# GpSimd's copies for a pair of heads ahead of its sums and splits, and the transfers in another order, in a fused attention and two-layer kernel

## Chip, core and metric

One core of a Trainium2 chip runs the whole kernel. The metric is the device time of one execution in microseconds.

## What is computed

The reference, cut to what matters (B, H, S, D = 2, 8, 768, 64; blocks of 32 keys, a window of 16):

```python
k_sum = k.reshape(B, H, nb, block, D).max(axis=3)
v_sum = v.reshape(B, H, nb, block, D).mean(axis=3)
scores_l = scale * q @ k^T            # kept where |i - j| < 16
scores_s = scale * q @ k_sum^T + log(32)
a = softmax(concat([scores_l, scores_s]))
x = a @ concat([v, v_sum])            # reshaped to 1536 x 512
h = x @ w_in                          # 512 -> 1024
solu = h * softmax(h); ln = layernorm(solu) * g_ln
x = ln @ w_out                        # 1024 -> 512
h = x @ w2_in                         # 512 -> 2048
out = where(h > 0, h, exp(min(h, 0)) - 1) @ w2_out
```

## The kernel before, in words

The kernel is written engine by engine, with semaphores between them; each engine runs its instructions in the order written, and every load is issued on the DMA queue of SyncE (SP).

**Attention stage.** The 16 heads go by pairs, 8 pairs of 6 units of 128 queries (48 units). For a pair, TensorE turns k (L881, `prep_k`) and q (L894, `prep_q`) with the identity; for a unit it computes scores against the neighbouring 96 keys (L910) and 24 block maxima (L918); VectorE adds the mask and finds the maximum (L694), ScalarE takes the exponential (L510), TensorE turns the probabilities (L927, L928, `turn_probs`), they are copied, and `attend` (L943) multiplies them by `vw`. Attend runs three units behind the scores, turning the probabilities two. After three attended units VectorE normalises them, and TensorE turns the result (L955) for the next stage.

`vw` holds three slots (VS = 3), one for each pair in turn. A slot has for each of 12 sub-blocks of 64 queries: 64 rows of v and 2 x 16 halo rows, and 24 rows of block means. The DMA queue loads the 64 own rows and part of the halo (`load_v`, L294 and L298). GpSimd copies the other halo rows from the neighbouring sub-block (`fill_halo`, L435), and spreads the block means over the 12 sub-blocks of both heads (`spread_means`, L444, two copies). The first attend of a pair waits for both.

The block means come from `vblocks` (two slots, four loads of 256 KB each, `load_vblocks`, L315): GpSimd adds halves until 64 columns are left (`block_means`, L408), and scales (L412); one call serves two pairs (four heads), so there are four calls (MEANS = 4). For the first one VectorE adds the first half (L728).

GpSimd also splits the weights of the first layer into high and low parts: `split_win` (L416, L418), four quarters of 512 KB, loaded by `load_win` (L319); and `split_wout`, four quarters, loaded by `load_wout` (L322). The first layer's products (L866 to L868) need all of win split, its second product (L1023 to L1025) all of wout.

k and q have four slots each (RAWS = 4; L277 and L284, two transfers of 192 KB per pair, one for each head, 64 numbers or 256 B a row; v is 384 KB and 8 KB). A load waits for its slot: v of pair n for attend group 6(n - 2) (that is, pair n - 3 attended), k and q for the turning of pair n - 4, vblocks c for the means of c - 2. A wait on SP holds all that is written behind it.

**Later stages.** x @ w_in row tile by row tile with softmax and layer norm (L748 to L808), then ln @ w_out; w2_in is loaded once the last scores are done, and w2_out after the first layer's products. The two products of the second layer (L866 to L868 and L1067 to L1069) fill the rest of the time from about 270 us on.

Of the kernel before, what the change touches and what calls it, by code (L numbers as in the profile page):

```python
# [25 lines left out]
P = 128  # L26


def fused_layers_kernel(nc, q, k, v, w_in, g_ln, w_out, w2_in, w2_out, out):
# [8 lines left out]
    PAIRS = B * H // 2  # L38
# [18 lines left out]
    KD = DM // P  # L57
# [11 lines left out]
    with ExitStack() as ctx:  # L69
# [57 lines left out]
        RING, VS = 4, 3  # L127

        HPM = P // BLOCK
        MEANS = B * H // HPM  # L130
# [32 lines left out]
        def sem(name):  # L163
            return ctx.enter_context(nc.semaphore(name))
# [11 lines left out]
        gcol_loaded = sem("gcol_loaded")  # L176
# [9 lines left out]
        win_hi_done, win_split, wout_hi_done, wout_split = (  # L186
            sem("win_hi_done"), sem("win_split"), sem("wout_hi_done"), sem("wout_split"))
# [19 lines left out]
        for g in range(GROUPS):  # L207
# [7 lines left out]
            else:  # L215
                ROWS_AND_TURNS[-1][1].extend(range(c, c + KF))
        assert [m for m, _ in ROWS_AND_TURNS] == list(range(TILES))
        assert [c for _, cs in ROWS_AND_TURNS for c in cs] == list(range(KF * GROUPS))
        TURNS = KF * GROUPS
        OUT_LAG = 2  # L220
# [34 lines left out]
        def v_landed(n):  # L255

            return 16 * (2 * (n // VS + 1) + (2 if n == PAIRS - 1 else 0))
# [11 lines left out]
        def _(sp):  # L269
            def pair_of_heads(x, n):  # L270
                return x[2 * n:2 * n + 2].rearrange("h (t p) d -> p t h d", p=P)

            def load_k(n):
                if n >= RAWS:
                    sp.wait_ge(kv_in_psum, n - RAWS + 1)
                for h in range(2):
                    sp.dma_start(kraw[:, n % RAWS, :, h * D:(h + 1) * D],  # L277
                                 pair_of_heads(kf, n)[:, :, h, :]).then_inc(k_loaded[n % RAWS], 16)

            def load_q(n):  # L280
                if n >= RAWS:
                    sp.wait_ge(q_in_psum, n - RAWS + 1)
                for h in range(2):
                    sp.dma_start(qraw[:, n % RAWS, :, h * D:(h + 1) * D],  # L284
                                 pair_of_heads(qf, n)[:, :, h, :]).then_inc(q_loaded[n % RAWS], 16)

            def load_v(n):

                s = n % VS
                if n < VS:  # L290
                    sp.wait_ge(zeros_ready, 1)
                else:
                    sp.wait_ge(attn_done, T * (n - VS + 1))
                sp.dma_start(vw[HALO:2 * HALO, s, :, 0, 0:D],  # L294
                             vf[2 * n:2 * n + 2, 0:HALO, :].rearrange("h i d -> i h d")).then_inc(v_loaded[s], 16)
                if n < PAIRS - 1:
                    rows = v_rows[2 * n * S + HALO:2 * (n + 1) * S + HALO, :].rearrange("(j i) d -> i j d", i=SUB)
                    sp.dma_start(vw[2 * HALO:LOCAL, s, :, :, 0:D].rearrange("i h j d -> i (h j) d"), rows).then_inc(v_loaded[s], 16)  # L298
                else:
                    rest = S - HALO - (SUBS - 1) * SUB  # L300
                    rows = v_rows[2 * n * S + HALO:(2 * n + 1) * S + HALO, :].rearrange("(j i) d -> i j d", i=SUB)
                    sp.dma_start(vw[2 * HALO:LOCAL, s, 0, :, 0:D], rows).then_inc(v_loaded[s], 16)
                    rows = vf[2 * n + 1, HALO:S - rest, :].rearrange("(j i) d -> i j d", i=SUB)
                    sp.dma_start(vw[2 * HALO:LOCAL, s, 1, 0:SUBS - 1, 0:D], rows).then_inc(v_loaded[s], 16)
                    sp.dma_start(vw[2 * HALO:2 * HALO + rest, s, 1, SUBS - 1, 0:D], vf[2 * n + 1, S - rest:S, :]
                                 ).then_inc(v_loaded[s], 16)

            def load_vblocks(c):

                if c >= 2:  # L310
                    sp.wait_ge(vmean_ready, c - 1)
                for i in range(HPM):
                    b0 = (HPM * c + i) * NB
                    b1 = min(b0 + QUAD, B * H * NB)
                    sp.dma_start(vblocks[i * QUAD:i * QUAD + b1 - b0, c % 2, :], v_blocks[b0:b1, :]  # L315
                                 ).then_inc(vblocks_loaded[c % 2], 16)

            def load_win(i):
                sp.dma_start(win_raw[:, i, :], w_in[i * P:(i + 1) * P, :]).then_inc(win_loaded[i], 16)  # L319

            def load_wout(i):
                sp.dma_start(wout_raw[:, 2 * i:2 * i + 2, :],  # L322
                             w_out[2 * i * P:(2 * i + 2) * P, :].rearrange("(k p) n -> p k n", p=P)
                             ).then_inc(wout_loaded[i], 16)
# [4 lines left out]
            load_k(1)  # L329
            load_v(0)  # L330
            load_q(1)
            load_v(1)
            load_vblocks(1)
            load_k(2)
            load_q(2)
            for n in range(PAIRS):
                if n + 2 < PAIRS:
                    load_v(n + 2)
                if n + 3 < PAIRS:
                    load_k(n + 3)  # L340
                    load_q(n + 3)
                if n < KD:
                    load_win(n)
                if 1 <= n and n + 1 < MEANS:
                    load_vblocks(n + 1)
                if n >= KD:
                    load_wout(n - KD)
                if n == KD:
                    sp.dma_start(gcol[:, :], g_ln.rearrange("(f p) -> p f", p=P),
                                 allow_slow_non_contiguous=True).then_inc(gcol_loaded, 16)  # L350

            sp.wait_ge(scores_in_psum, UNITS)
            sp.wait_ge(q_in_psum, PAIRS)
# [18 lines left out]
        def _(pool):  # L372
# [27 lines left out]
            def block_means(c):  # L400

                x, width = vblocks[:, c % 2, :], BLOCK * D // 2
                pool.wait_ge(vblocks_loaded[c % 2], 16 * HPM * (c // 2 + 1))
                if c == 0:
                    pool.wait_ge(first_half_summed, 1)
                    width //= 2
                while width >= D:
                    pool.tensor_tensor(x[:, 0:width], x[:, 0:width], x[:, width:2 * width], ALU.add).then_inc(vsum_step, 1)  # L408
                    vsteps[0] += 1
                    pool.wait_ge(vsum_step, vsteps[0])  # L410
                    width //= 2
                pool.tensor_scalar(vmean[:, c, :], x[:, 0:D], 1.0 / BLOCK, None, ALU.mult).then_inc(vmean_ready, 1)  # L412
                pool.wait_ge(vmean_ready, c + 1)

            def split(raw, hi, lo, hi_done, done, n):
                pool.tensor_copy(hi, raw).then_inc(hi_done, 1)  # L416
                pool.wait_ge(hi_done, n + 1)
                pool.tensor_tensor(lo, raw, hi.bitcast(F32), ALU.subtract).then_inc(done, 1)  # L418

            def split_win(i):  # L420
                pool.wait_ge(win_loaded[i], 16)
                split(win_raw[:, i, :], win_hi[:, i, :], win_lo[:, i, :], win_hi_done, win_split, i)
# [6 lines left out]
            def fill_halo(n):  # L429

                s = n % VS
                pool.wait_ge(v_loaded[s], v_landed(n))
                if n == 0:
                    pool.wait_ge(zeros_ready, 2)
                pool.tensor_copy(vw[0:2 * HALO, s, :, 1:SUBS, :],  # L435
                                 vw[SUB:LOCAL, s, :, 0:SUBS - 1, :]).then_inc(halo_filled, 1)
                pool.wait_ge(halo_filled, n + 1)

            def spread_means(n):

                s, c = n % VS, n // (HPM // 2)
                for h in range(2):
                    i = (2 * n + h) % HPM
                    pool.tensor_copy(vw[LOCAL:KEYS, s, h, :, 0:D],  # L444
                                     vmean[i * QUAD:i * QUAD + NB, c, None, :].broadcast_to([NB, SUBS, D])
                                     ).then_inc(means_spread, 1)
                    pool.wait_ge(means_spread, 2 * n + h + 1)

            block_means(0)
            fill_halo(0)  # L450
            spread_means(0)
            block_means(1)
            for n in range(PAIRS):
                if n < KD:
                    split_win(n)
                    pool.wait_ge(win_split, n + 1)
                if n + 1 < PAIRS:
                    fill_halo(n + 1)
                    spread_means(n + 1)
                if 1 <= n and n + 1 < MEANS:  # L460
                    block_means(n + 1)
            for i in range(KF // 2):
                split_wout(i)

            for g in range(GROUPS):
                pool.wait_ge(factors_ready, g + 1)
                for t in range(TG - pool_rows(g), TG):
                    i = (TG * g + t) % LNS
# [641 lines left out]
```

## Time and profile before

| | |
|---|---|
| median of 3 runs | 542.33 us (538.64 to 547.3) |
| profiled execution | 542.89 us, its span 541.1 us |
| mean granted TensorE clock | 0.972 of full speed |
| TensorE busy (matmuls) | 497.5 us, 92% of the span |
| VectorE, ScalarE, GpSimd busy | 232.1, 212.6, 127.5 us |
| moved by the DMA engines | 29.83 MB |

The span runs from the first to the last instruction of the profiled execution. Times in a timeline are microseconds from the span's start. A busy TensorE isn't TensorE at its peak, since its matmuls overlap and their ends are modelled.

### The profile page before, as it was taken

What the parts mean: (1) busy time and instruction counts of PE and PEld (TensorE: products, weight loads), DVE (VectorE), ACT (ScalarE), POOL (GpSimd) and SP (SyncE); (2) the same over time, 40 slices, a digit from 0 to 9 for tenths busy, and PEclk for the clock granted to TensorE, in tenths of its full rate; (3) what the DMA queues carried; (4) which work ended last, traced back from release to release, by engine and by line L of the source; (5) the groups of instructions that cost most, each with busy time, mean ns of one, the idle gap of its engine ahead of it and who ended that gap; (6) DMA issues with size and microseconds to landing.
All of it is one profiled execution on the core that took longest, in us unless ns stands there. A gap on an engine that the chain in (4) does not pass through costs nothing.

```text
span 541.1 us, 8560 instructions
## 1 busy us (share of the span) xinstructions
PE 497.5 (92%) x3312; PEld 417.2 (77%) x3312; DVE 232.1 (43%) x623; ACT 212.6 (39%) x433; POOL 127.5 (24%) x121
## 2 busy tenths in 40 slices
PE   3848669889699999999999999999999999999997
PEld 2636557667588989889988888888888888888886
DVE  2334525661686255355346555433333332323231
ACT  2434626671566254435464343323222223222222
POOL 2658396560012001102335545200000000000000
PEclk9987958999899999999999999999999999999999
DMA  9993936507000000008000000002000001000002
GB/s 187 216 233 89 232 97 129 149 13 302 0 0 2 0 1 1 1 1 310 2 0 1 0 1 1 1 0 79 0 1 0 1 0 68 10 0 0 0 0 78
DMA packets 45766, 29.83 MB, mean 55 GB/s; under 512 B 39596, under 2 KB 39596, under 8 KB 44716
## 3 DMA queue, kind: packets, MB, share of 16 engines
q1 hardware_dynamic: 45732, 29.37, 21.1%
q8 instruction: 23, 0.38, 0.3%
q14 instruction: 11, 0.09, 0.1%
HBM read 26.21 MB, written 3.15 MB: 54 GB/s over the span
## 4 chain that ended last, share of the span: by engine, by line
PE 81%; SPq 6%; POOL 3%; DVE 3%; DMA 3%; ACT 2%; issue 2%; POOLq 0%; DVEq 0%
PE bank L866 12%; PE bank L868 12%; PE bank L867 11%; PE bank L1069 8%; PE bank L1067 8%; PE bank L1068 8%; PE bank L1023 4%; PE bank L1025 4%; PE bank L1024 3%; PE bank L943 3%; SPq L284 3%; DMA win_raw<-in_w_in 3%; PE bank L910 2%; PE bank L1009 2%; SPq L277 1%
## 5 line engine op out<-in xcount | busy, mean ns | idle before, releaser
L627 ACT ACTIVATE ex<-bank 128x512 f32<-128x512 f32 x48 | 28.7, 598 | 127.9 <-PE bank L868 127.9
L868 PE MATMUL bank<-yt_lo,w2in_hi 128*128 (+1 forms) x192 | 74.7, 389 | 0.0
L867 PE MATMUL bank<-yt_hi,w2in_lo 128*128 (+1 forms) x192 | 74.7, 389 | 0.0
L1067 PE MATMUL bank<-w2out_hi,g_hi 128*128 128x512 f32 x192 | 74.7, 389 | 0.0
L1068 PE MATMUL bank<-w2out_lo,g_hi 128*128 128x512 f32 x192 | 74.7, 389 | 0.0
L866 PE MATMUL bank<-yt_hi,w2in_hi 128*128 (+1 forms) x192 | 74.7, 389 | 0.0
L1069 PE MATMUL bank<-w2out_hi,g_lo 128*128 128x512 f32 x192 | 74.7, 389 | 0.0
L844 DVE TENSOR_SCALAR ex<-ex 128x512 f32<-128x512 f32 x48 | 21.6, 450 | 116.4 <-ACT ex L627 116.4
L849 DVE TENSOR_TENSOR g_lo<-gf,g_hi 128x512 fp32r<-128x512 f32 x48 | 46.5, 969 | 35.9 <-ACT g_hi L635 35.9
L510 ACT ACTIVATE se<-se,nm 128x120 f32<-128x120 f32 x96 | 32.6, 387 | 49.7 <-DVE nm L694 49.7
L635 ACT ACTIVATE g_hi<-gf 128x512 fp32r<-128x512 f32 x48 | 30.3, 632 | 49.0 <-DVE gf L846 49.0
L1023 PE MATMUL bank<-lnt_hi,wout_hi 128*128 128x384 f32 x128 | 45.6, 356 | 1.2 <-DVE lnt_lo L803 1.2
L694 DVE CUSTOM_DVE_ANT_0 se<-bank,mask 128x120 f32<-128x120 f32 x96 | 23.1, 279 | 54.7 <-PE bank L918 54.7
L943 PE MATMUL bank<-vw,pt 120*64 120x65 f32 x384 | 24.8, 256 | 20.5 <-POOL vw L444 19.8
L866 PE MATMUL bank<-win_hi,xt_hi 128*128 128x512 f32 x96 | 38.9, 405 | 4.7 <-DVE su L764 4.7
L1025 PE MATMUL bank<-lnt_lo,wout_hi 128*128 128x384 f32 x128 | 43.1, 337 | 0.0
L1024 PE MATMUL bank<-lnt_hi,wout_lo 128*128 128x384 f32 x128 | 42.9, 335 | 0.0
L469 POOL TENSOR_SCALAR ln<-ln,st 128x1024 f32<-128x1024 f32 x10 | 12.5, 1260 | 125.1 <-DVE st L790 125.1
L1068 PEld LDWEIGHTS bank<-w2out_lo,g_hi 128*128 128x128 f32 x192 | 36.0, 188 | 7.6
L868 PEld LDWEIGHTS bank<-yt_lo,w2in_hi 128*128 128x128 f32 x192 | 36.0, 188 | 7.6
L1069 PEld LDWEIGHTS bank<-w2out_hi,g_lo 128*128 128x128 f32 x192 | 36.0, 188 | 7.5
L867 PEld LDWEIGHTS bank<-yt_hi,w2in_lo 128*128 128x128 f32 x192 | 36.0, 188 | 7.5
(102 smaller groups left out, 883.6 us busy)
## 6 DMA issues: line engine op xcount, KB each, us to landing
w2in_raw<-in_w_in SPq DMA_DIRECT2D x1, 4096.0 KB, 12.4
w2out_raw<-in_w_out SPq DMA_DIRECT2D x4, 1024.0 KB, 9.5
vblocks<-in_v SPq DMA_DIRECT2D x15, 256.0 KB, 6.1
kraw<-in_k SPq DMA_DIRECT2D x16, 192.0 KB, 4.8
qraw<-in_q SPq DMA_DIRECT2D x16, 192.0 KB, 4.4
out<-osb SPq DMA_DIRECT2D x12, 256.0 KB, 2.1
vw<-in_v SPq DMA_DIRECT2D x7, 384.0 KB, 5.0
win_raw<-in_w_in SPq DMA_DIRECT2D x4, 512.0 KB, 5.7
```

Of the source, the lines that this page charges most:

```text
L510: last = act.activation(se[:, s, h, :], se[:, s, h, :], ACT.Exp, scale=-1.0, bias=nm[:, s, h:h + 1])
L849: dve.tensor_tensor(g_lo[:, j % GS, :], gf[:, :], g_hi[:, j % GS, :].bitcast(F32), ALU.subtract).then_inc(glo_ready, 1)
L866: pe.matmul(acc, ah, bh, start=(i == 0), stop=False)
L867: pe.matmul(acc, al, bh, start=False, stop=False)
L868: last = pe.matmul(acc, ah, bl, start=False, stop=(i == n - 1))
L943: last = pe.matmul(psO[i * SUB:(i + 1) * SUB, c0:c0 + D1], pt[0:KEYS, u % 2, q0:q0 + SUB], vw[0:KEYS, v, h, 2 * t + i, :], start=True, sto ...
L1023: pe.matmul(dst, wout_hi[:, f, cols], lnt_hi[:, f, :], start=(f == 0), stop=False)
L1024: pe.matmul(dst, wout_lo[:, f, cols], lnt_hi[:, f, :], start=False, stop=False)
L1025: last = pe.matmul(dst, wout_hi[:, f, cols], lnt_lo[:, f, :], start=False, stop=(f == KF - 1))
L1067: pe.matmul(dst, g_hi[:, j % GS, cols], w2out_hi[:, j, :], start=(j == 0), stop=False)
L1068: pe.matmul(dst, g_hi[:, j % GS, cols], w2out_lo[:, j, :], start=False, stop=False)
L1069: last = pe.matmul(dst, g_lo[:, j % GS, cols], w2out_hi[:, j, :], start=False, stop=(j == KJ - 1))
```

## The change

GpSimd's program and the order of SP's loads are written out anew; no instruction of any other engine changes, and neither does the number or shape of any instruction or transfer.

```diff
             load_q(1)
+            load_k(2)
             load_v(1)
+            load_q(2)
             load_vblocks(1)
-            load_k(2)
-            load_q(2)
-            for n in range(PAIRS):
-                if n + 2 < PAIRS:
-                    load_v(n + 2)
-                if n + 3 < PAIRS:
-                    load_k(n + 3)
-                    load_q(n + 3)
-                if n < KD:
-                    load_win(n)
-                if 1 <= n and n + 1 < MEANS:
-                    load_vblocks(n + 1)
-                if n >= KD:
-                    load_wout(n - KD)
-                if n == KD:
-                    sp.dma_start(gcol[:, :], ...)
+            load_v(2)
+            load_k(3)
+            load_q(3)
+            load_win(0)
+            for n in range(VS, PAIRS):
+                load_v(n)
+                if n - 2 < KD:
+                    load_win(n - 2)
+                if n + 1 < PAIRS:
+                    load_k(n + 1)
+                    load_q(n + 1)
+                if n % 2 == 1 and n // 2 + 1 < MEANS:
+                    load_vblocks(n // 2 + 1)
+                if n >= 6:
+                    load_wout(n - 6)
+            sp.dma_start(gcol[:, :], ...)
+            load_wout(2)
+            load_wout(3)
...
+            def finish_v(n):
+                fill_halo(n)
+                spread_means(n)
+
+            def finish_win(i):
+                split_win(i)
+                pool.wait_ge(win_split, i + 1)
+
             block_means(0)
-            fill_halo(0)
-            spread_means(0)
+            finish_v(0)
+            finish_v(1)
             block_means(1)
-            for n in range(PAIRS):
-                if n < KD:
-                    split_win(n)
-                    pool.wait_ge(win_split, n + 1)
-                if n + 1 < PAIRS:
-                    fill_halo(n + 1)
-                    spread_means(n + 1)
-                if 1 <= n and n + 1 < MEANS:
-                    block_means(n + 1)
+            finish_v(2)
+            finish_win(0)
+            finish_win(1)
+            finish_v(3)
+            block_means(2)
+            finish_v(4)
+            finish_win(2)
+            finish_v(5)
+            block_means(3)
+            finish_v(6)
+            finish_win(3)
+            finish_v(7)
             for i in range(KF // 2):
                 split_wout(i)
```

## Rows read from the trace of the kernel before

**Rows 1.** The page: busy tenths and granted clock by slices; the chain by line.

```profile
PE   3848669889699999999999999999999999999997
...
PEclk9987958999899999999999999999999999999999
...
PE bank L866 12%; PE bank L868 12%; PE bank L867 11%; PE bank L1069 8%; PE bank L1067 8%; PE bank L1068 8%; PE bank L1023 4%; PE bank L1025 4%; PE bank L1024 3%; PE bank L943 3%; SPq L284 3%; DMA win_raw<-in_w_in 3%; PE bank L910 2%; PE bank L1009 2%; SPq L277 1%
```

**Rows 2.** Waits of TensorE, 0 to 130 us: total, times, longest.

```profile
PE bank L943 <- POOL vw L444: 19.8, 3, 9.3
PE bank L881 <- DMA kraw<-in_k: 7.3, 2, 4.8
```

**Rows 3.** Timeline of TensorE: start, duration, instructions, in brackets the idle time before.

```profile
20.16 0.70 PE L943 MATMUL bank<-vw,pt 120*64 120x65 f32 x8 [2.57 <-POOL vw L444]
...
32.84 0.27 PE L928 MATMUL bank<-ident,se 128*120 128x128 f32 x1
42.43 0.70 PE L943 MATMUL bank<-vw,pt 120*64 120x65 f32 x8 [9.32 <-POOL vw L444]
...
53.45 0.27 PE L928 MATMUL bank<-ident,se 128*120 128x128 f32 x1
53.66 0.45 PE L943 MATMUL bank<-vw,pt 120*64 120x65 f32 x8
...
71.76 0.70 PE L943 MATMUL bank<-vw,pt 120*64 120x65 f32 x8 [7.90 <-POOL vw L444]
...
86.37 0.45 PE L943 MATMUL bank<-vw,pt 120*64 120x65 f32 x8
...
96.50 0.45 PE L943 MATMUL bank<-vw,pt 120*64 120x65 f32 x8
...
104.92 0.39 PE L943 MATMUL bank<-vw,pt 120*64 120x65 f32 x5 [0.75 <-issue]
...
107.65 0.45 PE L943 MATMUL bank<-vw,pt 120*64 120x65 f32 x8
...
131.26 0.45 PE L943 MATMUL bank<-vw,pt 120*64 120x65 f32 x8
```

**Rows 4.** Timeline of GpSimd (POOL).

```profile
24.17 5.43 POOL L408 TENSOR_TENSOR vblocks<-vblocks 128x1024 f32<-128x1024 f32 x5 [4.16 <-DMA vblocks<-in_v]
...
35.52 1.04 POOL L416 CAST win_hi<-win_raw 128x1024 fp32r<-128x1024 f32 x1 [5.46 <-DMA win_raw<-in_w_in]
...
39.04 1.36 POOL L435 COPY vw<-vw 32x1430 f32<-32x1430 f32 x1
40.47 1.71 POOL L444 COPY vw<-vmean 24x768 f32<-24x768 f32 x2
43.09 1.04 POOL L416 CAST win_hi<-win_raw 128x1024 fp32r<-128x1024 f32 x1 [0.91 <-DMA win_raw<-in_w_in]
...
64.85 1.04 POOL L416 CAST win_hi<-win_raw 128x1024 fp32r<-128x1024 f32 x1 [9.10 <-DMA win_raw<-in_w_in]
...
157.61 1.74 POOL L469 TENSOR_SCALAR ln<-ln,st 128x1024 f32<-128x1024 f32 x1 [40.27 <-DVE st L790]
```

**Rows 5.** Stretches: busy time by engine, then granted clock, DMA share, GB/s.

```profile
0.00:24.17 24.17, 12.46 (x130) 9.81 (x134) 6.24 (x28) 7.98 (x17) 9.32 (x25) 1.00 1.07 200
24.17:35.52 11.35, 8.94 (x131) 6.89 (x130) 6.14 (x30) 5.88 (x16) 5.48 (x7) 1.00 1.03 229
35.52:43.09 7.57, 0.66 (x12) 0.57 (x12) 0.00 (x0) 0.00 (x0) 6.38 (x6) 0.59 1.06 236
...
52.50:70.30 17.80, 10.52 (x195) 8.01 (x195) 9.48 (x45) 9.48 (x26) 8.16 (x9) 0.92 1.02 203
```

**Rows 6.** Timeline of the DMA queue (SPq): v of pairs 3 and 4, win 2.

```profile
31.90 0.34 SPq L294 DMA_DIRECT2D vw<-in_v  x1
...
52.52 0.32 SPq L294 DMA_DIRECT2D vw<-in_v  x1
...
56.76 0.84 SPq L319 DMA_DIRECT2D win_raw<-in_w_in  x1
```

More of the change, by code:

```diff
@@ L331, in _ @@
             load_q(1)
+            load_k(2)
             load_v(1)
+            load_q(2)
             load_vblocks(1)
-            load_k(2)
-            load_q(2)
-            for n in range(PAIRS):
-                if n + 2 < PAIRS:
-                    load_v(n + 2)
-                if n + 3 < PAIRS:
-                    load_k(n + 3)
-                    load_q(n + 3)
-                if n < KD:
-                    load_win(n)
-                if 1 <= n and n + 1 < MEANS:
-                    load_vblocks(n + 1)
-                if n >= KD:
-                    load_wout(n - KD)
-                if n == KD:
-                    sp.dma_start(gcol[:, :], g_ln.rearrange("(f p) -> p f", p=P),
-                                 allow_slow_non_contiguous=True).then_inc(gcol_loaded, 16)
+            load_v(2)
[13 more added lines that the diff above has]
+                    load_wout(n - 6)
+            sp.dma_start(gcol[:, :], g_ln.rearrange("(f p) -> p f", p=P),
+                         allow_slow_non_contiguous=True).then_inc(gcol_loaded, 16)
+            load_wout(2)
+            load_wout(3)
             sp.wait_ge(scores_in_psum, UNITS)
```

## Prediction

> **What bounds the kernel now.** I read the page's slices first, then who waits for whom on TensorE, then the timelines of TensorE, GpSimd and the DMA queue side by side over the attention stage. In the slices TensorE is at 9 tenths nearly everywhere after the tenth slice (13.5 us each), and its holes lie in the third, fifth and sixth; the granted clock is low there or in the slice behind them, and in the chain by line the weight transfer win_raw has 3% of the span beside TensorE's own lines [rows 1]. So what can be won without touching the products lies in the first 130 us.
>
> There TensorE waits 19.8 us in three pieces for L444, the spread of block means, and 7.3 us in two for the first transfers of k [rows 2]. I number TensorE's attend groups (L943, eight matmuls) A0 to A47, six to a pair; A6, A12, A18 are the first of pairs 1, 2, 3. A0 starts at 20.16 after 2.57 us of waiting. A6 starts at 42.43 after 9.32 us; the probabilities for it were turned from 32.84. A18 starts at 71.76 after 7.90 us [rows 3]. GpSimd tells why. After the sums of vblocks 1 it waited 5.46 us for win_raw 0, split it, and only then copied halo and means of pair 1 (39.04 to 42.18), which had long been loadable. The same happened before A18: 9.10 us of waiting for win_raw 2, at 64.85 [rows 4]. The wait that ends last is thus a transfer of weights that the attention doesn't need, standing ahead of a 3.1 us copy in GpSimd's program. Its root is the DMA queue: its v transfer waits for attend groups, and one held it until 52.52, with win 2 issued behind it at 56.76 [rows 6].
>
> **The clock.** A matmul group of A takes 0.70 us just after each hole and 0.45 us later [rows 3]: the granted clock is at its 1.2 GHz level after a hole and comes back to 2.4. Six attend slots at full clock take 96.50 - 86.37 = 10.13 us (A24 to A30) [rows 3]. I take this as the price of a pair when nothing is late.
>
> **The change part by part.**
>
> GpSimd's program. The work is the same: no instruction is added or removed, only their order. So the first question is whether each copy of halo and means is ready before its pair. One pair of them costs 1.36 + 1.71 and some 0.1 of waits, 3.15 us; a sum of blocks 5.43 for the halvings, 6.0 us with the scaling and the waits (the first call is shorter, and the same in both); a split of win 3.5 us (35.52 to 39.04) [rows 4].
>
> The queue's program. The transfers are the same too, q and k still in two parts of 256 B rows each. Ahead of vblocks 1 now stand k 2 and q 2; from n = 3 on, win stands before k and q instead of behind them; vblocks 2 and 3 are issued at n = 3 and 5, the latter one v wait later. v of pair n still waits for the same attend group as before, as do k and q behind it. Nothing that waits for TensorE has moved ahead of something needed sooner.
>
> When things land. A pair of k or of q is 0.39 MB, of v 0.40, vblocks 1.05, a quarter of win 0.52. By 24.17 the DMA engines had moved 24.17 x 0.200 = 4.83 MB, when vblocks 1 landed with 4.47 MB ordered up to its end; at 35.52 and 43.09 win 0 and win 1 landed with 7.43 and 9.22 moved against 6.97 and 8.68 ordered [rows 4, 5]. So a transfer lands when about 0.45 MB more than its place in the order have moved. In the new order, at the same rates: v 1 (place 3.82) at 21.4, vblocks 1 (5.26) at 28.0, v 2 (5.66) at 29.8, win 0 at 35.4; v 3 is issued at 31.90 as before, being bound to A5 [rows 6], and lands at 37.2, win 1 at 39.4, vblocks 2 about 46.
>
> GpSimd against TensorE, then. Pair 1's copies start when v 1 is in, end at 24.6, and are needed at 33.05 (32.84 plus the 0.21 that lie between the rows at 53.45 and 53.66) [rows 3]. Sums of vblocks 1: 28.0 to 34.0. Pair 2's copies end 37.2, needed at A12. If nothing waits, A12 = 33.05 + 10.13 = 43.2, A18 = 53.3, A24 = 63.4, A30 = 73.6, A36 = 83.7. Win 0 and 1: to 44.2; pair 3: 47.4 against 53.3; sums 2: 53.3; pair 4: 56.5 against 63.4 (v 4, freed by A11 at 42, lands at about 50). Each has 6 us or more to spare.
>
> For the later transfers I take the 0.203 MB/us of the stretch 52.5 to 70.3 [rows 5], from 45.5 on when the queue would be empty. From v 4 to the end of vblocks 3 are 4.47 MB, plus 0.45: landed at 45.5 + 24.2 = 69.7. Sums 3 end 75.7 and pair 6 at 78.9, against 83.7: 4.8 us to spare, the tightest place. k 7 lands about 74 and is wanted about 80. win 3 and pair 7 follow, to 85.5 against 93.9, and the four splits of wout by about 100. These are moved behind nothing critical: in the trace of before GpSimd is done with wout so early that it then waits 40.27 us until 157.61 [rows 4], so 100 is early enough even for a stage that starts 23 us sooner.
>
> The sum. Hole before A6: 42.43 - 33.05 = 9.38. Half clock behind it: A6 to A12 took 53.66 - 42.43 = 11.23, less 10.13 = 1.10. A12 to A18: 71.76 - 53.66 = 18.10, less 10.13 = 7.97. A18 to A24: 86.37 - 71.76 = 14.61, less 10.13 = 4.48 [rows 3]. Together 22.9 us, of which 5.6 are clock. A0's wait and the two for k at the start stay: nothing ahead of them changes. What follows A30 is the same work, so it moves as a block. The profiled execution took 542.89 with a span of 541.1; 542.9 - 22.9 = **520.0**. The median of the runs is 542.33, 0.6 lower, within their spread of 538.64 to 547.3; I keep 520.
>
> Bounds of what the trace doesn't show. (a) Four pairs in a row without a hole: A30 to A36 took 107.65 - 96.50 = 11.15 us because of one gap of 0.75 that has no releaser but TensorE's own queue [rows 3]; with such a gap in each of four pairs the gain is 4 us smaller, 524. (b) After attention the slices show one more low slice of clock, a dip from 1.0 to about 0.87 over a slice of 13.5 us; were it spared, some 2 us more would be gained, and another 2 if the clock rose sooner after A0, 516. The nearest row for (a) is the neighbour of the one I use; I take none, since the other pairs at full clock ran without it.
>
> **The rivals.**
>
> *The transfers become the bound (R1).* Without holes TensorE uses a pair every 10.13 us, and a middle pair now orders 1.19 MB of k, q and v, 0.52 of weights and half of 1.05: 2.2 MB, at 0.203 some 11 us. The queue's lead therefore shrinks by 1 us a pair. Pair 6 is late if the rate falls under 4.92 / (83.7 - 9.2 - 45.5) = 0.170 MB/us. Against it: no stretch of rows 5 is below 0.200. At 0.150 the sums would start at 78.3, TensorE would wait 3.8 us, and the clock would drop once more, at the 4.5 us that it cost after A18: 528.
>
> *One copy is still late (R2).* If a transfer of win takes the 8.0 us from issue that win 2 took before (56.76 to some 64.8 [rows 4, 6]), win 1 lands at 41 rather than 39.4, and pair 3 still has 4 us. Only two such delays in the same stretch open a hole of a few us with its clock: 526. For it: sums of blocks still stand between the copies. Together with R1 I give these 523 to 532.
>
> *The clock stays low (R3), the slower side.* One mechanism: TensorE in this stage is a chain of short groups with gaps between them, and if the granted clock does not stay up without the old stops, every pair costs at least the 14.61 us of A18 to A24. A36 would come at 33.05 + 5 x 14.61 = 106.1, 1.5 before the old one; the stretch from there to the last attend group (131.26 - 107.65 = 23.6 us [rows 3]) would take 1.44 times as long, 10.4 more: about 552. It decides once more than half of the stage runs at 1.2 GHz. Against it: in the eighth to tenth slices the clock is at 9 while the same groups run without a hole [rows 1]. The Trainium skill, "TensorE: Matmul & The Clock Gate", section "A second HAM failure mode: psum-queue depth-cycling", describes just this: small idle times between matmul groups, often enough, make the clock swing between its two levels. By that rule 552 would be the time, by the rows 520; the rows from A24 to A36 speak against the rule here.
>
> *The order changes nothing (R4).* Halo and means could be late for v itself instead of for win. v 1 would have to land after 33; it was landed before the sums of vblocks 1 started at 24.17, so this needs 9 us of delay. Time 540.
>
> **How the numbers follow.** Forecast (with its bounds 516 to 524) 0.72; R1 and R2 together 0.18, at 523 to 532; R3 0.04; R4 0.03; the rest, 0.03, a gain larger than the bounds. The range 515 to 530 leaves out R3, R4 and the end of R1 and R2. Two per cent is about what a measurement of this kernel can tell from no change: 531.5. Below it lie the forecast, the larger gain and most of R1 and R2: 0.90; within 2%: 0.06; slower by more: 0.04, nearly all R3.
>
> **What the changed profile should show.** No wait of TensorE for L444 but the first, 2.6 us; A6 about 33, A12 43, A18 53, A30 74, and the last attend group about 108; the clock's slices at 9 from the third to the tenth; GpSimd waiting for vblocks 1 about 4 us after pair 1's copies, and no more than 1 or 2 us for win; the queue moving over 0.2 MB/us nearly without a break until 75. What would make me wrong: a wait of GpSimd for vblocks 3 that reaches A36, a wait for k in the later pairs, or groups of A at 0.70 us where there is no hole.

## The result, and the profile after

The changed kernel takes 517.29 us (median of 4, 516.36 to 517.76) against 544.51 of the kernel before (538.64 to 547.3): a ratio of 0.9532, interval 0.9443 to 0.9622. (The ratios, here and below, leave out executions more than 1.5% above the fastest of their kernel, like the one at 547.3; the medians don't.) Measured beside the experiments below, the kernel before had medians of 541.4 to 542.0. The changed kernel's profiled execution took 517.02 with a span of 515.2, against 542.89 and 541.1: 25.9 us less in the span.

The page's slices (each 12.9 us now), to be held against [rows 1]: the low slices of the attention stage are gone. The ninth, with 6 tenths, lies behind that stage and has its like in the kernel before (the eleventh). No digit of the granted clock is under 9.

```profile
PE   3798998969999999999999999999999999999997
...
PEclk9999999999999999999999999999999999999999
```

A 9 can hide a low clock, in two ways. At the start the row has 9 while groups of A still take 0.70 us (below): up to the clock's first rise the row reads as full, so there I go by the lengths of the groups. And behind the attention stage the dip that showed as an 8 in the kernel before is still there. TensorE waits 4.16 us in both, until 139.46 before and 113.63 now, and the clock is at 0.50 in the microseconds behind it; the slices only fall otherwise. These are stretches (columns as in [rows 5]), of the kernel before and of the changed one:

```profile
140.00:141.00 1.00, 1.00 (x4) 0.76 (x3) 0.96 (x5) 0.65 (x1) 0.00 (x0) 0.50 0.00 0
...
114.00:115.00 1.00, 1.00 (x3) 0.79 (x3) 0.96 (x4) 0.47 (x1) 0.00 (x0) 0.50 0.00 0
```

Waits of TensorE in its first 110 us, against [rows 2]: of the three waits for the spread of the means (L448 now) one is left, and the two for k at the start stand as they did.

```profile
PE bank L896 <- DMA kraw<-in_k: 7.3, 2, 4.6
...
PE bank L958 <- POOL vw L448: 2.4, 1, 2.4
```

Timeline of TensorE, attend groups (L958 now), against [rows 3]: A0, A2, A6, A12, A18, A24, A30, A36, A42 and A47.

```profile
19.83 0.70 PE L958 MATMUL bank<-vw,pt 120*64 120x65 f32 x8 [2.40 <-POOL vw L448]
...
24.83 0.46 PE L958 MATMUL bank<-vw,pt 120*64 120x65 f32 x8
...
31.06 0.45 PE L958 MATMUL bank<-vw,pt 120*64 120x65 f32 x8
...
41.23 0.45 PE L958 MATMUL bank<-vw,pt 120*64 120x65 f32 x8
...
51.98 0.45 PE L958 MATMUL bank<-vw,pt 120*64 120x65 f32 x8
...
61.60 0.45 PE L958 MATMUL bank<-vw,pt 120*64 120x65 f32 x8
...
71.73 0.45 PE L958 MATMUL bank<-vw,pt 120*64 120x65 f32 x8
...
81.86 0.45 PE L958 MATMUL bank<-vw,pt 120*64 120x65 f32 x8
...
91.85 0.45 PE L958 MATMUL bank<-vw,pt 120*64 120x65 f32 x8
...
105.44 0.45 PE L958 MATMUL bank<-vw,pt 120*64 120x65 f32 x8
```

A47 came at 105.44 instead of 131.26: 25.8 us sooner, and from there to the end 409.8 us pass in both kernels. The whole gain lies in the attention stage. By stretches between these rows (before, after):

| stretch | before | after | gain |
|---|---|---|---|
| start to A0 | 20.16 | 19.83 | 0.3 |
| A0 to A6 | 22.27 | 11.23 | 11.0 |
| A6 to A12 | 11.23 | 10.17 | 1.1 |
| A12 to A18 | 18.10 | 10.75 | 7.4 |
| A18 to A24 | 14.61 | 9.62 | 5.0 |
| A24 to A30 | 10.13 | 10.13 | 0.0 |
| A30 to A36 | 11.15 | 10.13 | 1.0 |
| A36 to A47 | 23.61 | 23.58 | 0.0 |

GpSimd's timeline, against [rows 4]. It shows the new order, the copies of pairs 1 to 4 before they are wanted, and the two long waits behind the first spread: 4.46 us for vblocks 1, and 6.32 us for vblocks 3, behind which pair 6's copies end at 79.00. No wait for win is left.

```profile
20.64 1.37 POOL L439 COPY vw<-vw 32x1430 f32<-32x1430 f32 x1 [0.95 <-DMA vw<-in_v]
22.07 1.71 POOL L448 COPY vw<-vmean 24x768 f32<-24x768 f32 x2
28.23 5.45 POOL L412 TENSOR_TENSOR vblocks<-vblocks 128x1024 f32<-128x1024 f32 x5 [4.46 <-DMA vblocks<-in_v]
...
35.63 1.71 POOL L448 COPY vw<-vmean 24x768 f32<-24x768 f32 x2
...
45.94 1.71 POOL L448 COPY vw<-vmean 24x768 f32<-24x768 f32 x2
...
55.12 1.71 POOL L448 COPY vw<-vmean 24x768 f32<-24x768 f32 x2
...
69.90 5.45 POOL L412 TENSOR_TENSOR vblocks<-vblocks 128x1024 f32<-128x1024 f32 x5 [6.32 <-DMA vblocks<-in_v]
...
77.29 1.71 POOL L448 COPY vw<-vmean 24x768 f32<-24x768 f32 x2
```

The stretch from 45.5 us, where the prediction began its reckoning, to the landing of vblocks 3, against the last row of [rows 5]: the DMA engines are busy throughout (share 1.02) at 208 GB/s.

```profile
45.50:69.80 24.30, 22.61 (x432) 17.71 (x427) 16.06 (x83) 18.46 (x50) 16.95 (x17) 1.00 1.02 208
```

The queue's v transfers of pairs 3 and 4, against [rows 6], are issued 1.3 and 10.4 us sooner, since the attend groups that free them come sooner.

```profile
30.60 0.43 SPq L294 DMA_DIRECT2D vw<-in_v  x1
...
42.10 0.43 SPq L294 DMA_DIRECT2D vw<-in_v  x1
```

### The profile page after: what moved, and what is told of

The parts are those of the page before. It is cut to its first block, busy times and chain, and to the rows that moved or that the text cites. A ratio compares the mean times of both kernels' runs of the same rounds, so it can differ in the third digit from the quotient of the medians.

```text
span 515.2 us, 8560 instructions
## 1 busy us (share of the span) xinstructions
PE 487.8 (95%) x3312; PEld 409.9 (80%) x3312; DVE 231.2 (45%) x623; ACT 212.2 (41%) x433; POOL 127.7 (25%) x121
## 4 chain that ended last, share of the span: by engine, by line
PE 88%; DVE 3%; issue 2%; ACT 2%; POOL 2%; DMA 1%; SPq 1%; DVEq 0%; POOLq 0%
PE bank L881 12%; PE bank L882 12%; PE bank L883 12%; PE bank L1082 8%; PE bank L1083 8%; PE bank L1084 8%; PE bank L1038 4%; PE bank L1040 4%; PE bank L1039 4%; PE bank L958 3%; PE bank L925 3%; PE bank L942 2%; PE bank L1024 2%; PE bank L970 1%; DMA vblocks<-in_v 1%
## 5 line engine op out<-in xcount | busy, mean ns | idle before, releaser
L1082 PEld LDWEIGHTS bank<-w2out_hi,g_hi 128*128 128x128 f32 x192 | 36.1, 188 | 7.5
L881 PEld LDWEIGHTS bank<-yt_hi,w2in_hi 128*128 128x128 f32 x192 | 36.0, 188 | 7.5
```

What stands on the lines that cost most here:

```text
L881: pe.matmul(acc, ah, bh, start=(i == 0), stop=False)
L1082: pe.matmul(dst, g_hi[:, j % GS, cols], w2out_hi[:, j, :], start=(j == 0), stop=False)
```

## The experiments

### Which of the two orders did it

Two kernels take one half of the change each. In the first, the block of loads is that of before; in the second, GpSimd's is.

```diff
 e1_gpsimd_only: the changed kernel
-            load_k(2)   ... the new order of loads
+            load_v(1)   ... the loads as before the change
 e2_queue_only: the kernel before
-            load_v(1)   ... its order of loads
+            load_k(2)   ... the changed one
```

Expected of the first:

> Only GpSimd's new order, with the transfers in the order of before. My theory (GpSimd's order was the cause; the transfers' order is worth little): every copy is still ready in time. Copies of pair 1 end near 23, sums 1 near 30, pair 2 near 33, win 0 and 1 near 46.5, pair 3 near 49.6 against A18 at 52, pair 4 near 58.7 against 61.6, the later ones earlier still. A47 at 105 to 106, the time within 1 us of the changed kernel: 516 to 519. Rival (both parts are needed): k, q or win come late in the old order, TensorE waits at pair 4 or 5 with its clock falling behind, 521 to 530.

It took 519.39 us against 541.98 of the kernel before, measured beside it: ratio 0.9589 (0.9519 to 0.9659). A47 came at 107.64. So GpSimd's order alone gives 22.6 us. The time is 0.4 over my theory's bound and A47 1.6 us later than it had; A0 came at 21.16, 1.3 us later than in the changed kernel. The rows of its GpSimd timeline run about 1 us behind the expected ones: pair 3's copies end at 50.6, a wait of 4.21 for win 1 stands before them, and TensorE doesn't wait for them.

```profile
43.92 1.04 POOL L416 CAST win_hi<-win_raw 128x1024 fp32r<-128x1024 f32 x1 [4.21 <-DMA win_raw<-in_w_in]
...
48.90 1.71 POOL L444 COPY vw<-vmean 24x768 f32<-24x768 f32 x2
```

Expected of the second:

> Only the new order of the transfers, with GpSimd's program of before. My theory: it makes things worse. Win 0 at 35.4 still stands ahead of pair 1's copies, so A6 stays near 42; and the sums of vblocks 3, loaded later now, stand ahead of win 3 and pair 4's copies: vblocks 3 lands near 77, sums to 83, win 3 to 86.5, pair 4's copies near 89.6, A24 near 90 after a hole of some 17 us, against 86.37 before. The hole before A18 shrinks to 0 to 3 us. Time 543 to 553. Rival (the transfers' order is what gave the gain, since weights come earlier): 525 to 535.

It took 547.59 us: ratio 1.0103 (1.0067 to 1.0139): about 1% slower than before, and clear of 1. TensorE's timeline has the three holes where they were expected: A6 as late as before, A18 with a small one, A24 with the long one (13.51 us where I had said some 17), as GpSimd waited 11.69 us for vblocks 3 and then split win 3 ahead of pair 4's copies.

```profile
41.91 0.70 PE L947 MATMUL bank<-vw,pt 120*64 120x65 f32 x8 [10.59 <-POOL vw L448]
...
65.45 0.45 PE L947 MATMUL bank<-vw,pt 120*64 120x65 f32 x8 [1.61 <-POOL vw L448]
...
89.73 0.70 PE L947 MATMUL bank<-vw,pt 120*64 120x65 f32 x8 [13.51 <-POOL vw L448]
```

GpSimd's timeline of the same kernel has the wait that leads to the last of them:

```profile
76.89 5.41 POOL L412 TENSOR_TENSOR vblocks<-vblocks 128x1024 f32<-128x1024 f32 x5 [11.69 <-DMA vblocks<-in_v]
```

The same order of transfers thus costs 5.6 us with one program on GpSimd and gains a little with the other: its cost is not its own, but that of what waits behind it.

### Is it the weights alone that stood in the way

```diff
 in GpSimd's loop of the kernel before
-                if n < KD:
-                    split_win(n)
-                    pool.wait_ge(win_split, n + 1)
                 if n + 1 < PAIRS:
                     fill_halo(n + 1)
                     spread_means(n + 1)
+                if n < KD:
+                    split_win(n)
+                    pool.wait_ge(win_split, n + 1)
```

> The kernel before, with one swap in GpSimd's loop: the copies of pair n + 1 stand ahead of the split of win n; sums of blocks and transfers as before. My theory: both holes shrink, but the sums, still ahead of the copies, leave small ones. Pair 1's copies end near 33.2 against A6 at 31 to 33 (hole up to 2 us), pair 3's near 55.6 against 53.3 (hole 2), pair 4's near 68 against 66 (hole 2), later ones in time. Time 523 to 530. Rival (the wait for win was all of it): within 1 us of the changed kernel, 516 to 519.

527.32 us, ratio 0.9702 (0.9639 to 0.9766): 14.7 us gained by one swap. The kernel with all of GpSimd's new order and the same transfers took 519.39, so the rest of that order, which takes the sums from in front of the copies too, is worth 7.9 us more. In TensorE's timeline the hole before A6 is 0.47 us, that before A18 4.62 (2 expected), and behind it the groups are at 0.70 us:

```profile
33.45 0.45 PE L943 MATMUL bank<-vw,pt 120*64 120x65 f32 x8 [0.47 <-POOL vw L444]
...
58.03 0.70 PE L943 MATMUL bank<-vw,pt 120*64 120x65 f32 x8 [4.62 <-POOL vw L444]
...
72.54 0.45 PE L943 MATMUL bank<-vw,pt 120*64 120x65 f32 x8
```

A18 to A24 takes 14.51 us. The hole that I had expected before A24 was not there: TensorE had been slow for so long that pair 4's copies, done at 70.5, caught up. So the losses of two pairs can't simply be added.

### The share of the clock

```diff
 the kernel before, attend, first group of pairs 1 and 3
+                    if n in (1, 3):
+                        pe.wait_ge(xn_ready, w)
+                    for _ in range({1: WARM1, 3: WARM3}.get(n, 0)):
+                        pe.matmul(psO[:, 2 * TG * D1:2 * TG * D1 + 96], ident[:, :], ident[:, 0:96], start=True, stop=True)
                     pe.wait_ge(halo_filled, n + 1)
```

> The kernel before, with 105 and 90 matmuls of 128 by 96 that nobody reads ahead of TensorE's two long waits for the copies of pairs 1 and 3 (and the wait for the normalised heads moved ahead of them). It tells the clock's share of the gain from the holes' own. My theory (5.6 us of the gain are half clock behind the holes): the holes stay in place, A6 near 42.4, but groups of A stay at 0.45 us; A6 to A12 and A18 to A24 take 10.1 instead of 11.2 and 14.6; time 5 to 6 us under before, 536 to 539. Rival (the slow groups behind a hole are caught up later because something else bounds them, or the clock falls nonetheless): within 2 us of before.

A miss of mine: 560.07 us, ratio 1.0321 (1.0258 to 1.0384). The fillers took 22.72 us where the hole was to be 9.3. I had taken 0.083 us for one from the pace of the transposes; it is 22.72 / 105 = 0.216. The trace says why. Each such product of 4-byte numbers stands in it as two matmuls (the 105 and 90 of the program add 390 to TensorE's 3312), while a transpose of the same numbers stands as one. The other half of the theory shows even here: behind the fillers A6 to A12 and A18 to A24 take 9.27 us each, at 0.45 us a group.

```profile
31.81 22.72 PE L939 MATMUL bank<-ident 128*128 128x96 f32 x202
```

With 40 and 33 of them:

> The keep-clock kernel again: the fillers took 0.216 us each, not the 0.083 I had reckoned with, so 105 and 90 of them were 22.7 and 20.3 us long and made the holes longer. Now 40 and 33, some 8.6 and 7.1 us. Theory (half clock behind the holes is 5 to 6 us of the gain): A6 near 42.4, A6 to A12 and A18 to A24 about 9.3 to 10.1, time 535 to 538. Rival (the clock's share is caught up): within 2 us of before.

Median 538.11 us against 541.41: ratio 0.9952 (0.9921 to 0.9983), 3.3 us. The profiled execution, at 535.0 the fastest of ten, shows the case in full: the fillers keep TensorE busy for 9.14 us, A6 stays late at 42.70, all groups are at 0.45, and the granted clock is 1.00 until TensorE's wait behind the attention stage.

```profile
33.63 9.14 PE L939 MATMUL bank<-ident 128*128 128x96 f32 x80
42.70 0.45 PE L948 MATMUL bank<-vw,pt 120*64 120x65 f32 x8
...
51.97 0.45 PE L948 MATMUL bank<-vw,pt 120*64 120x65 f32 x8
...
70.31 0.45 PE L948 MATMUL bank<-vw,pt 120*64 120x65 f32 x8
...
80.50 0.45 PE L948 MATMUL bank<-vw,pt 120*64 120x65 f32 x8 [0.86 <-POOL vw L445]
```

A6 to A12 takes 9.27 us there, less than the 10.13 of a steady pair, for which I take it that the other engines caught up in the hole. A18 to A24 takes 10.19, 4.4 less than before. So the clock's share is real: 1.96 + 4.42 = 6.4 us by these two stretches in this execution, the catching up included, and 3.3 in the median. The mean granted clock is 0.997 here and 0.981 to 0.993 in the other nine, so in them it was low for longer, somewhere; they have no trace. The wait itself is most of the loss, as reckoned.

### The price of a hole

Into the changed kernel, between `block_means(2)` and `finish_v(4)`, go 3 or 6 additions that nobody reads:

```diff
+            for _ in range(3):      # 6 in the second
+                pool.tensor_tensor(vblocks[:, 0, 0:1024], vblocks[:, 0, 1024:2048],
+                                   vblocks[:, 0, 1024:2048], ALU.add).then_inc(vsum_step, 1)
+                vsteps[0] += 1
+                pool.wait_ge(vsum_step, vsteps[0])
```

> The changed kernel with three more additions of 128 by 1024 numbers (2.37 us each, into a part of the block buffer that nobody reads any more) on GpSimd between the third sums and pair 4's copies: 7.1 us. It measures the slack there and the price of a short hole. In the changed kernel pair 4's copies ended at 56.8 and A24 came at 61.6, so 4.8 us are free. Theory: a hole of 2.3 to 2.6 us before A24, no fall of the clock behind so short a hole, time 2.5 us over the changed kernel, 519 to 520. Rival (a short hole costs clock too): 522 to 525.

Median 520.06 us, 518.44 to 524.9: the median is as the theory had it, the highest as the rival. The trace is of that highest one. A24 waits 3.37 us, and a granted clock of 0.50 follows:

```profile
64.71 0.70 PE L963 MATMUL bank<-vw,pt 120*64 120x65 f32 x8 [3.37 <-POOL vw L448]
...
79.40 0.45 PE L963 MATMUL bank<-vw,pt 120*64 120x65 f32 x8
```

A24 to A30 takes 14.69 us, 4.6 more than a steady pair: the clock costs more than the hole. The executions of 518.44 and 519.14 us had a mean clock of 0.997, that of the changed kernel's profiled one, so theirs didn't fall at this place. Whether they had the same hole and chance decided, or a shorter one, isn't shown, as they have no trace. (The additions took 1.89 us each, and the sums of vblocks 2 had started 1.7 us later than in the changed kernel. Together they put the end of pair 4's copies from 56.8 to 64.5, 7.6 us, while A24 came 3.1 us later: 4.5 us of it were free, near the 4.8 that I had reckoned with.)

> The same with six additions, 14.3 us: 9.5 us beyond the slack. Theory (a long hole costs itself and half clock behind it, 1 to 5 us as in the kernel before): a hole of 9.5 us before A24, groups of A at 0.70 us behind it, 11 to 15 us over the changed kernel, 528 to 532. Rival (waiting engines catch up behind the hole, as A6 to A12 did in 9.27 us when fillers kept the clock): 526 to 527.

Median 528.48 us, 528.2 to 529.73: 11.4 over the 517.1 of the changed kernel as measured for the next section, within the theory. Pair 4's copies ended at 69.3 and A24 came at 69.58, 8.0 us behind the changed kernel's 61.60, A30 at 84.22 (14.64 later). The wait next to A24 reads only 4.74 us, for behind a gap of 1.33, at 51.46, the clock had already fallen once, and slow groups used up a part of the hole:

```profile
51.46 0.49 PE L975 MATMUL bank<-ident,xn 128*128 128x128 f32 x3 [1.33 <-DVE xn L735]
...
69.58 0.70 PE L963 MATMUL bank<-vw,pt 120*64 120x65 f32 x8 [4.74 <-POOL vw L448]
```

Its stretch behind that gap has a granted clock of 0.58:

```profile
52.00:60.00 8.00, 8.00 (x105) 6.25 (x105) 3.36 (x19) 4.37 (x11) 7.44 (x8) 0.58 0.98 231
```

### What the transfers' order is worth

The changed kernel and the one with the old transfers again, side by side on one chip:

> The changed kernel itself, on the same chip as the next two, so that one can be held against the other. Both theories: 516 to 518, the last attend group about 105.

517.12 us (516.04 to 517.72), ratio 0.9563 (0.9529 to 0.9598).

> GpSimd's new order with the old transfers, beside the changed kernel on the same chip. In the first run it was 2.1 us over the changed kernel's median of another chip job; there 1.7 us of it was a wait of TensorE for q and 1.3 us a later A0, before which nothing differs. Theory A (the transfers' order is worth the wait for q, 1 to 2 us, and A0 was chance): 1 to 2.5 us above the changed kernel here, with the wait for q again. Theory B (worth nothing): within 0.5 us.

Median 521.72 us, ratio 0.9637 (0.9583 to 0.9692): 4.6 above it, or 3.3 without the highest execution, 526.46; more than either theory had. The intervals of the ratios just overlap, but five of the six executions lie above all six of the changed kernel. A part of the theory fell with the traces. The wait of 1.7 us for q, of which it spoke, was that for the first q of all, ahead of A0, where the two orders are still the same; behind A0 neither profiled execution has one. What there is instead are gaps of about 1 us with no releaser:

```profile
50.64 0.49 PE L966 MATMUL bank<-ident,xn 128*128 128x128 f32 x3 [0.81 <-issue]
...
65.86 0.30 PE L929 MATMUL bank<-ks,qt 64*64 64x24 f32 x5 [1.19 <-issue]
```

Of the 1.96 us by which this profiled execution is longer than the changed kernel's beside it, 0.9 come after A47, where the two programs are the same: 410.7 us against 409.8, and over 112 to 120 us, behind TensorE's wait of 4.16, its granted clock is 0.57 on average against 0.79 in the changed kernel's first profile. That dip was longer by chance.

To see which part of the order matters, each half of it was undone in the changed kernel:

```diff
 e11_queue_later_part
-            load_k(2); load_v(1); load_q(2); load_vblocks(1)
+            load_v(1); load_vblocks(1); load_k(2); load_q(2)
 e12_queue_early_part: from v of pair 3 on
-            v n, win n-2, k n+1, q n+1; vblocks 3 with n = 5
+            v n, k n+1, q n+1, win n-2; vblocks 3 with n = 4
```

> The changed kernel, with the early transfers (through v of pair 2) in the old order: v 1, vblocks 1, k 2, q 2. Only the later part of the queue's order is new. In the last call the old order as a whole gave 521.7 with a spread of 517 to 526, the new one 517.1 with 516 to 518. Theory A (it is the later part, win ahead of k and q and vblocks 3 later, that steadies the time): 516 to 518.5 here. Theory B (it is k 2 and q 2 early): 519 to 523.

518.81 us (517.99 to 521.35), ratio 0.9592 (0.9564 to 0.9619): 0.3 over Theory A's bound, and just under Theory B's. In its profiled execution (517.99) A47 came at 104.94, 0.5 sooner than in the changed kernel, so the attention stage lost nothing there; the dip behind A47 was the longer one.

> The other half: k 2 and q 2 early, the later transfers in the old order (k and q ahead of win, vblocks 3 one v wait sooner). Theory A: 519 to 523, as widely spread as with the whole old order. Theory B: 516 to 518.5.

523.89 us, 517.37 to 528.54, ratio 0.9625 (0.9579 to 0.9671). The pair speaks for Theory A, that the later part of the order is what steadies the time, though the intervals of the ratios overlap. The profiled execution (525.11 us) shows how one becomes long. A gap of 2.36 us without a releaser stands in pair 2, and A12 to A18 then takes 16.33 us:

```profile
42.48 0.45 PE L958 MATMUL bank<-vw,pt 120*64 120x65 f32 x8
...
47.37 0.37 PE L942 MATMUL bank<-ident,se 128*120 128x128 f32 x1 [2.36 <-issue]
...
47.89 0.70 PE L958 MATMUL bank<-vw,pt 120*64 120x65 f32 x8
...
58.81 0.45 PE L958 MATMUL bank<-vw,pt 120*64 120x65 f32 x8
```

In the stretches the clock falls within the gap (0.74 as its mean) and is at 0.50 behind it; the groups of A are at 0.70 us up to 55.77, and 55 to 58 has a mean of 0.77. That makes some 10 us at the lower level. The columns are as in [rows 5].

```profile
45.00:47.30 2.30, 0.01 (x1) 0.00 (x0) 0.00 (x0) 0.18 (x1) 2.24 (x2) 0.74 1.27 199
47.30:50.00 2.70, 2.63 (x32) 1.79 (x33) 0.58 (x5) 1.22 (x3) 2.50 (x4) 0.50 0.64 128
50.00:55.00 5.00, 5.00 (x59) 3.99 (x58) 2.71 (x13) 2.45 (x8) 4.60 (x6) 0.50 1.01 234
```

What the gap waits for isn't shown. But the DMA rows hold a trail. The page has two queues that it calls "instruction", q8 and q14; q8 moves 23 packets of 0.02 MB in a whole execution. Some gaps of TensorE in the attention stage stand in some traces and not in the others, and aren't waits for the spread of the means. From A0 to 110 us all traces together have twelve of 0.45 us or more: the 2.36 above and one of 0.46 in the same trace, 0.81 and 1.19 above, 0.51 in the changed kernel, 0.75 in the kernel before, 1.63 and 0.45 in the first half-change, 0.81 in the second, 0.79 in the next experiment, 0.57 in the kernel with 40 and 33 fillers, 1.33 in the one with six additions. All twelve end 2.3 to 3.1 us after a packet of q8 has started, and six of them stand at the same place of the program, the transposes of xn just ahead of A18. For the 0.45, which ended at 59.65, the packet shows in the stretch from 56.8 to 57.0:

```profile
q8 instruction: 1, 0.02, 40.6%
```

Most packets of q8 are followed by no gap. This fits code that arrives late, behind data that fill the DMA engines, but no run here took the data away, so it stays argued. Why the old later order should bring such gaps more often stays open too.

### One step further

What TensorE's first wait ends on is GpSimd's chain of sums, halo and spread. ScalarE is idle for 1.5 us between 15.7 and 17.9 (0.43 and 1.09), and can take the halo copy of pair 0, which GpSimd then leaves out:

```diff
 in ScalarE's loop, behind copy_k(1)
+                if u == 1:
+                    act.wait_ge(v_loaded[0], v_landed(0))
+                    act.wait_ge(zeros_ready, 2)
+                    act.activation(vw[0:2 * HALO, 0, :, 1:SUBS, :], vw[SUB:LOCAL, 0, :, 0:SUBS - 1, :],
+                                   ACT.Copy).then_inc(halo0_filled, 1)
```

> The changed kernel, with the halo copy of pair 0 done by ScalarE behind its first copy of k, so that GpSimd goes from the first means to their spreading. Theory (what TensorE's first wait ends on is GpSimd's chain of sums, halo and spread): A0 about 1.3 us sooner, wait 1.1 instead of 2.4, and all behind it moves along: 1 to 1.4 us under the changed kernel, 515.0 to 516.5. Rival (the clock's rise or the next wait eats it, or ScalarE's exponentials come later): no difference.

517.67 us (515.29 to 522.75) beside 517.12: no difference that counts, and a wider spread. The mechanism is there, A0 comes at 18.50, 1.3 us sooner. But in this execution (519.65 us) the clock was still low when it had risen in the changed kernel: the sixth group still took 0.67 us, and A6 came at 32.52 instead of 31.06.

```profile
18.50 0.70 PE L962 MATMUL bank<-vw,pt 120*64 120x65 f32 x8 [1.08 <-POOL vw L446]
...
30.68 0.67 PE L962 MATMUL bank<-vw,pt 120*64 120x65 f32 x8
32.52 0.45 PE L962 MATMUL bank<-vw,pt 120*64 120x65 f32 x8
```

That need not come of the earlier A0: with the 40 and 33 fillers A0 came at 19.64 and the groups were as slow for as long. Three of the six executions, from 515.29 to 517.00, are as fast as the changed kernel or faster; whether the clock rose early in them isn't shown, as they have no trace. No version of these beats the changed kernel.

## Why the prediction was right

The forecast was 520.0, in the range 515 to 530; the time is 517.3.

*What bounds the kernel.* Right, and tested from both sides: taking the split of win from in front of the copies gives 14.7 us, moving the copies ahead of the later sums as well gives 22.6, both with the old transfers; the new transfers without GpSimd's new order lose 5.6.

*GpSimd against TensorE.* The reckoned times (what TensorE's grid allowed aside) came within 0.9 us everywhere: pair 1's copies ended at 23.8 (24.6 reckoned), sums 1 at 34.2 (34.0), pair 2 at 37.3 (37.2), win 0 and 1 at 44.4 (44.2), pair 3 at 47.7 (47.4), pair 4 at 56.8 (56.5), vblocks 3 landed at 69.9 (69.7), pair 6's copies at 79.0 (78.9), pair 7's at 85.8 (85.5). The rate taken for the later transfers, 0.203 MB/us, is near the 0.208 measured. One landing was off by more: vblocks 2 came at 47.4 rather than about 46, which cost nothing, since GpSimd was ready for it only at 47.7. And "6 us or more to spare" was too much: pairs 2, 3 and 4 had 3.9, 4.3 and 4.8 us, as TensorE's grid ran some 2 us ahead of the reckoned one.

*The sum.* The mechanism held and the terms of the second hole were sized well: 7.97 + 4.48 = 12.45 against 7.35 + 4.99 = 12.34 measured; so was the clock behind the first, 1.10 against 1.1. Too small was the term of the hole before A6: A0 to A6 got shorter by 11.0 us rather than 9.4, because the clock rose at A2 (24.83) and not at A4. That is luck of the two profiled executions and no work of the change: among kernels that are the same up to there, the groups were at 0.70 us up to A1 (the 105 fillers), A3 (before, and the swap) and A5 (the 40 fillers). A0 itself came 0.3 sooner, and the gap of 0.75 us between A30 and A36, which I had left in the block that moves, was gone, 1.0 us. The clock's rise and the gap are in the bounds that I gave, the one in (b), the other the reverse of (a). Together these make up the 2.9 us by which the span shrank more than forecast (25.9 against 22.9); by medians measured side by side the gain is 24.3. The other part of (b) didn't come: the low clock behind the attention stage wasn't spared, though its digit went from 8 to 9, and A47 to the end took 409.8 us in both.

*The rivals.* R1: pair 6 had 81.86 - 79.00 = 2.9 us to spare rather than 4.8, since TensorE came 1.8 us sooner; the transfers are not the bound, but they are near. R2 didn't come true in either profile of the changed kernel. R3: the clock stayed up through the whole stage with gaps of up to 0.9 us in each pair, so the Trainium skill's "TensorE: Matmul & The Clock Gate", section "A second HAM failure mode: psum-queue depth-cycling", doesn't describe this stage as it stands; yet the clock fell in or just behind gaps of 1.33, 1.61 and 2.36 us in three experiments, so R3 was closer than I thought. I had costed clock only behind holes of 8 us.

*The transfers.* I took the new order for harmless and let GpSimd's do all the work. That holds for most of the gain: GpSimd's order alone gave 22.6 us in one measurement and 541.41 - 521.72 = 19.7 in another, beside which both together gave 24.3. The transfers' order is worth the rest, some 2 to 5 us: nine of the ten executions without it lie above all ten with it. It is worth that by steadiness, which no term of my sum had, and whose cause stays open.

## What to carry to other kernels

On an engine that works for others in program order, put what the next consumer waits for ahead of anything that itself waits for a transfer, and check it pair by pair with the consumer's grid, not by busy time: GpSimd was 24% busy here, and its order cost some 20 us. An order of transfers has no price of its own: the same one gave 2 to 5 us with the fitting program behind it and took 5.6 with the other. Ask of each stop of TensorE what it costs in clock as well, since stops of 2.36 and 3.37 us cost 3.8 and 4.6 more here, where the clock fell.

## What the runs showed of the hardware

- In one execution the clock fell within a gap of 2.36 us in TensorE's work, between stretches at full clock, and stayed at the lower of its two levels for some 10 us; that cost 3.8 us beyond the gap (16.33 - 10.13 - 2.36). A gap of 3.37 cost 4.6 in one execution; others of the same kernel kept a mean clock of 0.997, their gaps unseen. Behind gaps of 1.33 (six additions) and 1.61 (new transfers alone, where a group 2.7 us later takes 0.70 us) it fell too; behind one of 1.63, in the first half-change, it didn't (A18 to A24 took 9.96 us). Gaps of 0.8 to 0.9, one a pair, left it at 1.00.
- The same wait can be followed by dips of different lengths. Behind the 4.16 us after the attention stage, 112 to 120 us has a mean clock of 0.79 in the changed kernel and 0.57 in three of its variants. With the short dip A47 to the end takes 409.7 to 410.0 us, with the long one 410.6 to 411.2.
- How long the clock stays low at the start varies: one group of A at 0.70 us with three additions, two in the changed kernel, four in the kernel before, five and most of a sixth with the halo copy on ScalarE and with 40 fillers.
- A product of 4-byte numbers stands in the trace as two matmuls, a transpose with the identity as one. So a matmul of 128 by 96 takes 0.216 us by its pace here, where six transposes of 128 by 128 take 0.85.
- Twelve gaps of TensorE that only some traces have (0.45 to 2.36 us) all end 2.3 to 3.1 us after a packet on the instruction queue q8 has started.
- GpSimd's addition of 128 by 1024 takes 1.89 us where its two inputs are the same part of the buffer and the output another, against 2.37 in the sums of blocks, where the first input is also the output. Which of the two counts isn't shown.
